# Attention's apply started from the copy that lands first, the sums' small steps moved between the masks, and two key blocks of the mix issued around the last apply

## What is computed

```python
# attention, batch 4, 8 heads, 512 local and 32 global tokens, head size 64
s_g = scale * q_g @ k_all.T                 # 32 global queries see all 544 keys
out_g = softmax(s_g) @ v_all
s_l = [scale * q_l @ k_g.T, where(|i - j| <= 32, scale * q_l @ k_l.T, -1e9)]
out_l = softmax(s_l) @ [v_g; v_l]           # softmax: e / (sum(e) + 1e-9)
x = concat(out_g, out_l)                    # 4 x 544 rows of 512
# channel mix: x_prev is x shifted by one row
k = max((mu_k * x + (1 - mu_k) * x_prev) @ w_k, 0)
x2 = sigmoid(xr @ w_r) * (k * k @ w_v)
# then a routed layer: each row is sent to one of 8 experts, out = p * relu(x2 @ w1[e]) @ w2[e]
```

## Time and profile before

| | |
|---|---|
| median of 3 runs | 700.87 us (700.58 to 702.92) |
| the profiled execution | 700.96 us |
| its span | 699.3 us |
| PE, PEld busy | 637.5 us (91%), 527.5 us (75%) |
| DVE, ACT, POOL busy | 366.6 us (52%), 281.6 us (40%), 185.2 us (26%) |
| chain that ended last | PE 81%, DVE 7%, ACT 5%, issue 4% |
| attention | first scores at 7.14 us, first matmul of the mix at 134.25 us |

### The profile page before, as it was taken

The page is one execution under the profiler, slowest core; times in us unless marked ns, Lnnn a source line. Parts: engine busy times, 40 slices in busy tenths (PEclk is TensorE's granted clock), DMA queues, the critical chain, the costliest instruction groups (busy, mean ns, idle before and its releaser), DMA issues.

```text
span 699.3 us, 15184 instructions
## 1 busy us (share of the span) xinstructions
PE 637.5 (91%) x4666; PEld 527.5 (75%) x4667; DVE 366.6 (52%) x920; ACT 281.6 (40%) x615; POOL 185.2 (26%) x263
## 2 busy tenths in 40 slices
PE   7899999899999999999999703999999999999994
PEld 6787777777887787789788502887888888888883
DVE  3677778594445626445434295649253353353531
ACT  4666678444313422332321140547243252262521
POOL 5676762200000000000000064235515215124140
PEclk9999999999999999999999855999999999999997
DMA  9878871000100010010010283658526135145000
GB/s 326 314 250 280 279 256 61 2 0 1 46 15 1 19 43 0 0 45 16 1 46 1 79 312 119 207 171 304 205 81 217 60 95 215 45 134 182 10 26 3
DMA packets 29204, 78.09 MB, mean 112 GB/s; under 512 B 4330, under 2 KB 7146, under 8 KB 29168
## 3 DMA queue, kind: packets, MB, share of 16 engines
q1 hardware_dynamic: 24368, 63.47, 26.1%
q0 software_dynamic: 4800, 14.16, 5.8%
HBM read 69.49 MB, written 9.70 MB: 113 GB/s over the span
## 4 chain that ended last, share of the span: by engine, by line
PE 81%; DVE 7%; ACT 5%; issue 4%; DMA 1%; POOL 0%; DVEq 0%; ACTq 0%; POOLq 0%
PE banks L723 22%; PE banks L725 21%; PE banks L724 21%; ACT prob L1343 3%; PE banks L869 3%; PE banks L742 2%; PE banks L668 1%; DMA xg<-x_rows,rows_in 1%; PE banks L844 1%; PE banks L630 1%; PE banks L615 1%; ACT probT L1353 1%; PE banks L674 1%; PE banks L734 1%; PE banks L686 1%
## 5 line engine op out<-in xcount | busy, mean ns | idle before, releaser
L518 POOL TENSOR_TENSOR we_lo<-we_raw,we_hi 128x1024 f32 (+1 forms) x18 | 50.4, 2822 | 319.8 <-ACT we_hi L1462 319.8
L1316 DVE TENSOR_SCALAR hid<-banks 128x512 f32<-128x512 f32 x40 | 27.7, 692 | 94.2 <-PE banks L725 92.8
L1343 ACT ACTIVATE prob<-neg,negmax 128x160 f32<-128x160 f32 (+1 forms) x136 | 59.2, 437 | 38.6 <-DVE negmax L929 27.4
L1462 ACT ACTIVATE we_hi<-we_raw 128x1024 f32 (+1 forms) x64 | 63.8, 1051 | 12.8 <-issue 8.1
L723 PE MATMUL banks<-we_hi,hid_hi 128*128 x160 | 66.8, 418 | 1.4 <-DVE hid_lo L1321 1.4
L723 PE MATMUL banks<-we_hi,xg_hi 128*128 x160 | 65.8, 411 | 1.7 <-DVE xg_lo L1287 1.7
L724 PE MATMUL banks<-we_lo,xg_hi 128*128 x160 | 63.8, 399 | 0.0
L725 PE MATMUL banks<-we_hi,xg_lo 128*128 x160 | 63.7, 398 | 0.0
L725 PE MATMUL banks<-we_hi,hid_lo 128*128 x160 | 63.1, 395 | 0.0
L724 PE MATMUL banks<-we_lo,hid_hi 128*128 x160 | 63.1, 394 | 0.0
L723 PE MATMUL banks<-mix_hi,wm_hi 128*128 128x512 f32 (+2 forms) x160 | 58.6, 366 | 0.5 <-DVE k_raw L1063 0.3
(11 more groups left out here) (215 smaller groups left out, 1400.6 us busy)
## 6 DMA issues: line engine op xcount, KB each, us to landing
we_raw<-in_w_e SPq DMA_DIRECT2D x64, 512.0 KB, 4.4
qk<-in_qk_t SPq DMA_DIRECT2D x32, 448.0 KB, 6.1
vw<-in_v_t SPq DMA_DIRECT2D x32, 256.0 KB, 4.5
w_raw<-in_w_mix POOLq DMA_DIRECT2D x20, 256.0 KB, 4.5
x_rows<-x SPq DMA_DIRECT2D x17, 256.0 KB, 2.0
vz<-in_v_z SPq DMA_DIRECT2D x8, 128.0 KB, 2.9
vx<-in_v_x SPq DMA_DIRECT2D x8, 96.0 KB, 5.1
qg<-in_qg_t SPq DMA_DIRECT2D x8, 64.0 KB, 6.8
```

What stands on the lines that cost most here:

```text
L518: return pool.tensor_tensor(we_lo[:, buf, 2 * j:2 * j + 2, :].rearrange("p x a b -> p x (a b)"), we_raw[:, j, :].unsqueeze(1), we_hi[:, bu ...
L1316: dve.tensor_scalar(hid[:, D * h:D * (h + 1)], ps_h[:, h, :], 0.0, None, ALU.max).then_inc(hid_ready, 1)
L1343: act.activation(prob[:, t % 2, c], neg[:, c], ACT.Exp, scale=-1.0, bias=negmax[:, t % 2, k:k + 1], accum_out=rsum[:, t % 2, k:k + 1]).the ...
L1462: act.activation(we_hi[:, buf, 2 * j:2 * j + 2, :].rearrange("p x a b -> p x (a b)"), we_raw[:, j, :].unsqueeze(1), ACT.Copy).then_inc(we_ ...
```

## The change

Four edits are made together. (1) `apply` waits for VectorE's half of `probT` only, does the matmuls that need just that half (the part of the global keys for all four heads, then the window of heads 2 and 3), and waits for ScalarE's half ahead of those of heads 0 and 1. (2) `invert_sums` is split into `guard_sums` (the addition) and `invert_sums` (the reciprocal); in a step whose own unit is local they come behind the first and the second mask; in a step with a global unit they stay ahead of its mask. (3) The twelve matmuls of key block 0 of the mix are issued ahead of the last `apply`, those of block 1 behind it. (4) The warm-up is 20 transposes and then 18 small matmuls with a rounded copy of the identity, which ScalarE makes.

```diff
-WARM_UP = 30
+WARM_UP = 20
...
-                pe.wait_ge(probT_a, n + 1)
                 pe.wait_ge(probT_b, n + 1)
...
+                    for pair in (1, 0):
+                        if pair == 0:
+                            pe.wait_ge(probT_a, n + 1)
                         for blk in range(2):
                             for h in range(2):
...
+                    for cs in ((2, 3, 4), (0, 1)):
+                        if cs[0] == 0:
+                            pe.wait_ge(probT_a, n + 1)
+                        for pair in range(2):
+                            for c in cs:
...
+            pe.wait_ge(ident_rounded, 1)
+            for n in (P, P // 2, P // 4):
+                for _ in range(6):
+                    pe.matmul(banks[:, 7, 0:n], ident_r[:], ident_r[:, 0:n], start=True, stop=True)
...
+            def keys_part(g, tiles, f):
+                half, col = divmod(P * f, D)
+                for c in range(DC):
+                    mm = three_pass(ps_k[:, f % 2, 0:P * tiles], [a[:, HALVES * c + half, col:col + P] for a in wm],
+                                    [a[0][:, c, 0:P * tiles] for a in (mix_hi, mix_lo)], c == 0, c == DC - 1)
+                mm.then_inc(k_summed, 1)
+
+            apply(B - 1, UNITS - 2)
+            turn(B - 1, UNITS - 1)
+
+            pe.wait_ge(masked, heads_done(B - 1, UNITS - 1))
+            pe.wait_ge(mix_lo_ready, DC + 2)
+            pe.wait_ge(wm_lo_ready, MIX_CHUNKS)
+            keys_part(0, GT, 0)
+            apply(B - 1, UNITS - 1)
+            keys_part(0, GT, 1)
...
+                        if last and k == 0:
+                            guard_sums(*last)
+                        if last and k == 1:
+                            invert_sums(*last)
...
-                if behind(b, t, 1):
-                    invert_sums(*behind(b, t, 1))
-                mask_scores(b, t)
+                last = behind(b, t, 1)
+                if last and unit(t)[1] is None:
+                    guard_sums(*last)
+                    invert_sums(*last)
+                mask_scores(b, t, last)
...
+            act.wait_ge(ident_made, 2)
+            act.activation(ident_r[:], ident[:], ACT.Copy).then_inc(ident_rounded, 1)
```

More of the change, by code:

```diff
@@ L668, in apply @@
                             pe.matmul(o[DH * h:DH * (h + 1), P * pair:P * (pair + 1)], vz[i][:, 2 * pair + h, :],
-                                      pt(HEADS), start=True, stop=False)
+                                      pt(HEADS), start=(pair == 0), stop=False)
+                    for pair in (1, 0):
+                        if pair == 0:
+                            pe.wait_ge(probT_a, n + 1)
                         for blk in range(2):
@@ L674, in apply @@
                                 mm = pe.matmul(o[DH * h:DH * (h + 1), P * pair + QB * blk:P * pair + QB * (blk + 1)],
-                                               vw[i][:, j, v0:v0 + DH], pt(k, QB * blk, QB), start=False, stop=(blk == 1))
+                                               vw[i][:, j, v0:v0 + DH], pt(k, QB * blk, QB), start=False, stop=(pair == 0 and blk == 1))
                 else:
@@ L678, in apply @@
                     rows = P - WIN
[L679 to L693, removed]
+                    for cs in ((2, 3, 4), (0, 1)):
[3 more added lines that the diff above has]
+                            for c in cs:
+                                for h in range(2):
+                                    k = 2 * pair + h
+                                    od = o[DH * h:DH * (h + 1), SG * pair:SG * (pair + 1)]
+                                    v0 = HEADS * DH + DH * k
+                                    if c < JT - 1:
+                                        mm = pe.matmul(od, vw[i][:, c, v0:v0 + DH], pt(c, SG * k, SG),
+                                                       start=(c == 2 and pair == 0),
+                                                       stop=(c == 1 and pair == 1))
+                                    elif c < JT:
+                                        mm = pe.matmul(od, vw[i][0:rows, c, v0:v0 + DH], pt(c, SG * k, SG, rows),
+                                                       start=False, stop=False)
+                                    else:
+                                        mm = pe.matmul(od, vx[i][:, DH * k:DH * (k + 1)], pt(c, SG * k, SG, rows),
+                                                       start=False, stop=False)
@@ L751, in mix_group @@
                 pe.wait_ge(mix_lo_ready, 2 * DC * g + DC + 2)
-                for f in range(FC):
+                for f in range(2 if first_group(g) else 0, FC):
                     pe.wait_ge(k_squared, FC * g + f + 1)
[L755 to L759, removed]
+                    keys_part(g, tiles, f)
                     if f < 2 and not first_group(g):
@@ L912, in _, with mask_scores @@
             dve.wait_ge(mask_made, 8)
-            def mask_scores(b, t):
+            def mask_scores(b, t, last):
                 _, j = unit(t)
                 s = ps_s[:, t % 2]
-                ng = neg
                 dve.wait_ge(scored, UNITS * b + t + 1)
@@ L928, in mask_scores, with sums, guard_sums, invert_sums @@
                         pair, h = divmod(k, 2)
-                        dve.tensor_tensor_reduce(ng[:, KW * k:KW * (k + 1)], s[:, h, KW * pair:KW * (pair + 1)],
+                        dve.tensor_tensor_reduce(neg[:, KW * k:KW * (k + 1)], s[:, h, KW * pair:KW * (pair + 1)],
                                                  mask[:, m, :], -SCALE, HUGE, ALU.add, ALU.min,
                                                  negmax[:, t % 2, k:k + 1]).then_inc(masked, 1)
+                        if last and k == 0:
+                            guard_sums(*last)
+                        if last and k == 1:
+                            invert_sums(*last)
                 else:
-                    dve.tensor_scalar(ng[:, 0:SL + SG], s.rearrange("p a b -> p (a b)")[:, 0:SL + SG], -SCALE, HUGE,
+                    dve.tensor_scalar(neg[:, 0:SL + SG], s.rearrange("p a b -> p (a b)")[:, 0:SL + SG], -SCALE, HUGE,
                                       ALU.mult, ALU.min, accum_out=negmax[:, t % 2, 0:1]).then_inc(masked, 1)
-            def invert_sums(b, t):
+            def sums(b, t):
                 w = 1 if unit(t)[1] is None else HEADS
-                rs = rsum[:, t % 2, 0:w]
+                return w, rsum[:, t % 2, 0:w], UNITS * b + t
+            def guard_sums(b, t):
+                w, rs, n = sums(b, t)
                 dve.wait_ge(exped, heads_done(b, t + 1) if t + 1 < UNITS else heads_done(b + 1, 0))
                 dve.tensor_tensor(rs, rs, eps[:, 0:w], ALU.add).then_inc(summed, 1)
-                dve.wait_ge(summed, UNITS * b + t + 1)
+            def invert_sums(b, t):
+                w, rs, n = sums(b, t)
+                dve.wait_ge(summed, n + 1)
                 if not (first_batch(b) and t < 2):
-                    dve.wait_ge(spread, UNITS * b + t - 1)
+                    dve.wait_ge(spread, n - 1)
                 dve.reciprocal(rinv[:, t % 2, 0:w], rs).then_inc(inverted, 1)
```

6 lines of the change are left out of this document (3 added, 3 removed).

## The result

The change makes the kernel slower: median 705.02 us (703.55 to 708.43, 12 runs) against 700.88 us (699.33 to 702.92, 12 runs), ratio 1.0055, 95% interval 1.0041 to 1.0069. The profiled execution took 703.89 us with a span of 702.2, so 2.9 more than that of before.

What follows compares the result with a forecast made beforehand. TensorE's chain was taken to bound the kernel, zigzagging between all four engines in attention. First units +0.8, units 8 to 32 +2.4, last seven +0.7, key blocks -0.8, warm-up 0: 704.1 us from 700.96; range 698.5 to 708.5.

Steps and rivals of the forecast that it cites:

- `rb` becomes the wait: Local attention steps: TensorE's `rb` transposes wait for GpSimd in place of ScalarE's `probT`; 702.8 to 706.5 us, chance 0.52.
- Reciprocal at s+1.65, `rb` at s+2.35, step 3.10: Local steps, counted from s, the start of a step's scores: reciprocal was s+0.77, transposes s+2.07, step 2.82.
- rival D: VectorE neighbours overlap less, so full lengths count: reciprocal at s+1.84, +4.7 us, 708 to 709; chance 0.10.
- GpSimd's backlog: Behind two weight pieces and a load, transposes come 0.31 late once more, in five of 24 steps: +1.5 us.
- Units 8 to 32, +2.4: 24 attention steps: 73.05 us from step lengths, with GpSimd's term 74.5 to 74.7 against 72.28.
- First eight units, +0.8: Start of attention, same rate of 0.10 a step; unit 7's pause might swallow it, so -0.6 to +1.4 us.
- Last seven units, +0.7: Attention from 103.90 to 126.24, same rate a step; earlier first mask and later reciprocal balance as elsewhere.
- The key blocks, -0.8: Before the last apply: key block 0 fills TensorE's gaps of 0.94 and 0.30, less 0.40; first square stays hidden.
- The warm-up, 0: Kernel start: ten fewer transposes take off 1.07 us, 18 small matmuls add 1.1; bounds -0.5 and +0.8.
- Sum: Whole kernel: +0.8 + 2.4 + 0.7 - 0.8 + 0 = +3.1 us on 700.96, so 704.1.

Runs made afterwards that it cites:

- moving the pieces: Changed kernel with GpSimd's two-piece weight steps put behind other units, six of them behind an early reciprocal: 704.16 us, ratio 1.0031 to the kernel before.
- edit 1 alone: Kernel before with only apply going by VectorE's half of `probT` first: 697.98 us, ratio 0.9941.
- edit 2 alone: Kernel before with only the addition behind the first mask and the reciprocal behind the second in local steps: 705.56 us, ratio 1.0053.
- edit 4 alone: Kernel before with only the new warm-up, 20 transposes and 18 small matmuls: 701.71 us, ratio 0.9996.
- the twelve transposes: Kernel before with apply by VectorE's half first, key block 0 ahead of the last apply, and 12 warm-up transposes in place of 30: 696.78 us, ratio 0.9920.
- edits 1 and 3: Kernel before with apply by VectorE's half first and key block 0 ahead of the last apply, 30 warm-up transposes: 697.43 us, ratio 0.9935.

## Why the prediction was right, step by step

- **`rb` becomes the wait.** Right: 23 waits of 10.1 us against three of 1.2. Putting only the sums back takes 8.8 us off.
- **Reciprocal at s+1.65, `rb` at s+2.35, step 3.10.** The reciprocal was at s+1.66 and the transposes at s+2.35. Two small errors cancel in the first: the mask came at s+1.09 where I took s+1.04, and from there to the reciprocal it was 0.57 where I took 0.61. The step is 3.04: the tail of the turn from there is 0.69, where I took 0.75 from a step in which the transposes came without a wait. By full lengths (rival D) the second mask would have come 0.16 behind the addition's start; it came 0.08 behind it (62.49 to 62.57). Rival D's rule was that of "VectorE: DVE Perf Modes", "The DRAIN you can't avoid" in the Trainium skill; the trace agrees with the section's own exception, that an instruction which is not held starts earlier.
- **GpSimd's backlog.** I had five steps of the 24; there are five at 3.34 to 3.52 (units 13, 16, 19, 22 and 28), and moving the pieces moved most of them. Not all five are the late reciprocal's: with the sums put back the steps of units 19 and 28 are still 3.51 and 3.35, and before the change that of unit 19 was 3.43 already. In the step of unit 19 the addition runs beside a weight piece of GpSimd and is held by it (last section), which my working did not have.
- **Units 8 to 32, +2.4.** Measured +2.05; the steps of 3.04 in place of 3.10 account for most of the difference.
- **First eight units, +0.8.** From unit 0 to 8: 25.19 against 24.48, +0.7. The pause of 1.61 in unit 7's scores is not in this profile, so without it the loss was 2.3, and the term's agreement is partly luck. The fall of the granted clock in units 1 and 2, which the profile of before does not have, is part of these 2.3, and no run takes the two apart.
- **Last seven units, +0.7.** Wrong in size and sign: 22.22 against 22.34, -0.1. The expectation that these balance as elsewhere missed the step of unit 36, which was 3.85 before and is 3.19: there ScalarE's half was very late, and edit 1 took it back (3.20 with edit 1 alone, 3.50 with edit 2 alone), which pays for the other steps.
- **The key blocks, -0.8.** Measured -1.05 in the changed kernel's trace and -0.99 alone; what I had set aside for handing over (0.40) was 0.35 idle less some 0.2 of other gaps.
- **The warm-up, 0.** The mis-sized one: +0.85 to the first scores, at the very edge of what I had set (0.8; by my own numbers it would have been 0.86). I had taken 1.1 for the small matmuls because they have fewer columns; they took 2.20, 0.11 apart with 32 columns as with 128, which is the pace of a late transpose; the ten transposes less took off 1.19. Whether this reaches the end is not shown: edit 4 alone measured 0.3 us less than before, with an interval from 1.3 less to 0.8 more.
- **Sum.** +0.85 + 0.70 + 2.05 - 0.12 - 1.05 = +2.4 at key block 2, and 0.5 behind it. That stretch is the same work in all twelve profiles and takes 558.9 to 561.0 us in them, so 0.5 is scatter. It is 2.9 in all in this profile, against the forecast +3.1; the medians differ by 4.1, with 2.9 to 4.8 as the interval. That the sum came so close is partly luck: the warm-up was 0.85 over its term and the last seven units 0.8 under theirs. The mechanism and its main term (units 8 to 32) came out as worked out, and that was not luck.

## What to carry to other kernels

An instruction that stands in a hole of its engine is free, and moving it out of the hole costs more than its length when it feeds a chain over another engine: here 0.88 of delay on a reciprocal of 0.18, behind a wait for scores that it didn't need. Before moving a small producer, count the slack from it to its last consumer in steps where nothing is late, and compare that with the delay. The slack was 0.6 before and 0.5 with edit 1, which lets the consumer come earlier. Up to the slack nothing happens (reciprocal at s+1.28 in place of s+0.77); beyond it each further tenth is paid in each step. And measure edits of one change apart: edit 1 was worth 4 us, and could show none of it beside edit 2.

## What was not expected of the hardware

- A stream of matmuls with a 128x128 rounded float32 weight load each ran at 0.11 us apiece, for 128, 64 and 32 columns alike (each load 192 ns), and the late transposes of the plain float32 identity ran at 0.11 as well. So shrinking the columns bought no time.
- TensorE's first instructions come 0.21 apart, and at some moment the distance halves to 0.11, for transposes and for small matmuls alike. The moment differs from execution to execution: it lies between 4.3 and 7.3 us in the ten profiles with the longer warm-ups, and has not come when the twelve transposes are over. Between 5.2 and 5.8 us, of the same thirty transposes, it has passed with edits 1 and 3 and has not with edit 1 alone; and between 6.0 and 6.6 the small matmuls of the run with the sums ahead of the masks are still slow, 0.21 apart:

```profile
L706 PEld LDWEIGHTS banks<-ident x7: 139/140/142, 5.1 to 5.8; 128*128 128x128 f32 x7
...
L706 PEld LDWEIGHTS banks<-ident x4: 226/226/226, 5.1 to 5.8; 128*128 128x128 f32 x4
...
L712 PEld LDWEIGHTS banks<-ident_r x4: 333/336/338, 5.8 to 6.4; 128*128 128x128 f32 x4
```

  This is why the first scores of otherwise like kernels started anywhere within 1.3 us (6.4 to 7.7) behind thirty transposes that all began at 1.65. The granted clock of the profile is 1.00 on both sides of the change, so it does not show it; what sets the moment is not shown.
- VectorE's addition of `rsum` and `eps`, both in SBUF, is 0.15 to 0.17 long wherever no GpSimd instruction runs beside it (189 times between 9 and 128 us in the twelve profiles). Beside one it can be as long as 1.28, and of the 131 that are longer than 0.2, 126 end within 0.05 of the end of GpSimd's copy, rounding or subtraction. In the step of unit 19, with the sums ahead of the masks:

```profile
63.09 1.27 POOL L443 TENSOR_TENSOR wm_lo<-w_raw,wm_hi 128x512 fp32r<-128x512 f32 x1
63.78 0.60 DVE L963 TENSOR_TENSOR rsum<-rsum,eps 128x4 f32<-128x4 f32 x1
```

  The reciprocal, which reads one tile, stays at 0.15 to 0.18 beside the same instructions.
- Pauses of 1 to 2.3 us that no semaphore explains came at different units in different profiles (1.61 in unit 7's scores before, 2.27 ahead of unit 12's with edit 1 alone), and so did stretches at the lower granted clock. A term of 1 us at the start of this kernel can't be read from one profile.
